# Projecting the last two row blocks of each group tile of tokens by tile of tokens, in a fused attention and two-mixture kernel

## The reference

```
def _moe2_ref(x, domain_probs, w1, w2):      # x 1536 x 512, w1 4 x 512 x 1024, w2 4 x 1024 x 512
    p = domain_probs / (domain_probs.sum(-1, keepdims=True) + 1e-09)
    out = np.zeros((N, D), dtype=np.float32)
    for e in range(E):
        h = np.maximum(x @ w1[e], 0.0)
        out += p[:, e:e + 1] * (h @ w2[e])
    return out.astype(np.float32)
```

## Time and profile before

| | |
|---|---|
| median of 3 runs | 909.2 us (908.07 to 913.29) |
| the profiled execution's own time | 910.04 us |
| its span, first to last instruction | 908.2 us |
| TensorE busy | 860.9 us, 95% |
| weight loads (beside the matmuls) | 695.1 us, 77% |
| VectorE, GpSimd, ScalarE busy | 300.3, 288.8, 221.3 us |
| second mixture, from its first hidden matmul to the end | 378.3 to 908.2 us |
| mean granted TensorE clock over the span | 0.987 of full speed |

### The profile page before, as it was taken

How to read it: one execution, slowest core, us unless ns; L and a number is a source line. 1 busy time by engine, 2 the same in 40 slices (tenths; PEclk the granted TensorE clock), 3 DMA queues, 4 the chain that set the end, 5 groups by cost and what they waited for, 6 DMA issues and landing times.

```text
span 908.2 us, 12900 instructions
## 1 busy us (share of the span) xinstructions
PE 860.9 (95%) x4433; PEld 695.1 (77%) x4434; DVE 300.3 (33%) x776; ACT 221.3 (24%) x476; POOL 288.8 (32%) x162
## 2 busy tenths in 40 slices
PE   7999945999999999999999999999999999999998
PEld 5666623788888788788888888888888888888886
DVE  6777770444444443223121212121212121211212
ACT  4878750033333323311111111111111111111010
POOL 4462613057777778630000650000830001400000
PEclk9999976999999999999999999999999999999999
DMA  6899623146666667620000230000320000001001
GB/s 246 265 315 342 221 78 140 31 124 213 205 204 205 195 220 220 174 94 1 1 0 0 70 116 0 0 0 0 115 71 0 0 0 0 1 0 46 29 17 46
DMA packets 33075, 90.96 MB, mean 100 GB/s; under 512 B 4232, under 2 KB 4616, under 8 KB 33040
## 3 DMA queue, kind: packets, MB, share of 16 engines
q1 hardware_dynamic: 23056, 54.86, 18.1%
q10 hardware_dynamic: 8064, 29.36, 10.6%
q0 software_dynamic: 1920, 6.29, 2.2%
HBM read 72.67 MB, written 17.83 MB: 100 GB/s over the span
## 4 chain that ended last, share of the span: by engine, by line
PE 84%; DMA 8%; DVE 3%; issue 2%; POOL 2%; SPq 1%; ACT 1%; DVEq 0%; ACTq 0%
PE ps L1209 29%; PE ps L1196 29%; PE ps L1153 10%; PE ps L1135 7%; DMA win<-qkv 3%; DMA xg<-x_sorted 3%; PE ps L1008 2%; PE ps L1034 2%; PE ps L1020 2%; POOL x_sorted L473 1%; PE ps L1143 1%; PE ps L1125 1%; PE ps L979 1%; PE ps L1048 1%; ACT arena L528 1%
## 5 line engine op out<-in xcount | busy, mean ns | idle before, releaser
L1209 PE MATMUL ps<-ring,h 128*128 128x512 f32 x1152 | 275.9, 390 | 0.0
L1196 PE MATMUL ps<-ring 128*128 (+1 forms) x864 | 256.4, 389 | 0.0
L278 POOL TENSOR_TENSOR ring<-raw,ring 128x1024 fp32r<-128x1024 f32 x96 | 227.9, 2403 | 84.0 <-ACT ring L273 81.1
L1209 PEld LDWEIGHTS ps<-ring,h 128*128 128x128 f32 x1152 | 215.6, 188 | 44.6
L1196 PEld LDWEIGHTS ps<-ring 128*128 128x128 f32 x864 | 162.1, 188 | 34.0 <-DVE x2b L940 0.2
L947 DVE SCALAR_TENSOR_TENSOR h<-ps,h 128x512 fp32r<-128x512 f32 x96 | 66.3, 691 | 366.3 <-ACT h L597 366.3
L597 ACT ACTIVATE h<-ps 128x512 fp32r<-128x512 f32 x96 | 57.6, 600 | 427.3 <-PE ps L1196 427.3
L273 POOL CAST ring<-raw 128x1024 fp32r<-128x1024 f32 x36 | 38.0, 1055 | 374.8 <-PE ps L1196 320.3
L1196 PE MATMUL ps<-x2b,ring 128*128 (+1 forms) x288 | 112.0, 389 | 0.0
L273 ACT CAST ring<-raw 128x1024 fp32r<-128x1024 f32 x60 | 62.2, 1051 | 176.9 <-PE ps L1153 116.7
L1135 PE MATMUL ps<-ring,xT 128*128 x384 | 91.8, 395 | 0.6 <-DVE xT L900 0.6
(11 more groups left out here) (116 smaller groups left out, 490.2 us busy)
## 6 DMA issues: line engine op xcount, KB each, us to landing
raw<-wts ACTq DMA_DIRECT2D x56, 512.0 KB, 4.2
raw<-wts SPq DMA_DIRECT2D x40, 512.0 KB, 3.8
win<-qkv SPq DMA_DIRECT2D x32, 320.0 KB, 4.1
x_sorted<-ring SPq DMA_DIRECT2D x20, 256.0 KB, 4.9
xg<-x_sorted SPq DMA_DIRECT2D x17, 256.0 KB, 3.4
y_sorted<-yrow SPq DMA_DIRECT2D x16, 256.0 KB, 4.0
win<-qkv SPq DMA_DIRECT2D x8, 384.0 KB, 6.3
result<-xrow SPq DMA_DIRECT2D x12, 256.0 KB, 2.1
```

Source lines behind the costliest of these rows:

```text
L278: nc.gpsimd.tensor_tensor(w_part(u, 1)[:, q * CW:q * CW + CW], raw[:, q, :], w_part(u, 0)[:, q * CW:q * CW + CW].bitcast(F32), ALU.subtrac ...
L1196: ins = nc.tensor.matmul(ps[:, 4 + f % 2, :], w_part(u1, wp)[:, k * F + f * P:k * F + f * P + P], x2T(xp, k)[:, bass.ds(g * 512, 512)], st ...
L1209: ins = nc.tensor.matmul(ps[:, t, :], h2[:, f % 2, hp_, t * P:t * P + P], w_part(u1 + 1, wp)[:, f * DM:f * DM + DM], start=(f == 0 and n = ...
```

## The change

In each group the row blocks 6 and 7 are no longer projected one after the other. project(f) runs for f = 0 to 5 alone, and a new function, finish(), follows the loop. It waits for the split of all 8 blocks and for the fourth quarter of w2. Then, for each tile of tokens, it runs the 3 matmuls of block 6 and the 3 of block 7, and signals y2_ready. hid_used of block 6 is signalled with the last tile. The numbers of matmuls, their operands and the banks are the same. In the loop's passes f = 6 and 7 what is left is hidden(7) and, in the first group, the turning of tiles 10 and 11. No other engine's program is changed.

```diff
--- before.py
+++ after.py
@@ -1214,13 +1214,29 @@
                     if f < KF - 1:
                         ins.then_inc(hid_used, 1)
 
+                def finish():
+
+                    pe.wait_ge(hid_split, n0 + KF)
+                    pe.wait_ge(split_done, 4 * (u1 + 1) + KF // 2)
+                    for t in range(4):
+                        for f in (KF - 2, KF - 1):
+                            for n, (hp_, wp) in enumerate(((0, 0), (0, 1), (1, 0))):
+                                ins = nc.tensor.matmul(ps[:, t, :], h2[:, f % 2, hp_, t * P:t * P + P],
+                                                       w_part(u1 + 1, wp)[:, f * DM:f * DM + DM],
+                                                       start=False, stop=(f == KF - 1 and n == 2))
+                            if f == KF - 2 and t == 3:
+                                ins.then_inc(hid_used, 1)
+                        ins.then_inc(y2_ready, 1)
+
                 hidden(0)
                 for f in range(KF):
                     if f + 1 < KF:
                         hidden(f + 1)
                     if beside:
                         beside(f)
-                    project(f)
+                    if f < KF - 2:
+                        project(f)
+                finish()
 
             for t in range(4):
                 turn_x2(t)
```

## The result

| | before | changed |
|---|---|---|
| median of 4 runs | 910.38 us (908.07 to 913.29) | 933.17 us (931.05 to 936.0) |
| ratio, 95% interval | | 1.0247 (1.0218 to 1.0276) |
| profiled execution, its span | 910.04, 908.2 us | 936.0, 934.2 us |
| TensorE busy | 860.9 us | 867.0 us |
| first hidden matmul of the second mixture | 378.28 us | 382.76 us |

The kernel is 2.5% slower, as forecast. The profiled execution is the slowest of its four runs. Its span is 26.0 us longer, and the first thing to do is to divide that: up to the first hidden matmul, where nothing was changed, it is 382.76 - 378.28 = 4.5 us behind; from there on it is (934.2 - 382.76) - (908.2 - 378.28) = 21.5 us longer. Only the 21.5 belong to the change.

What follows compares the result with a forecast made beforehand. The prediction took gapless TensorE matmuls at full clock to bound the second mixture's stage. Eleven groups at 1.77 us plus 1.93 for the first gave 21.4 us, so 930.6 us, range 927.4 to 936.0.

Steps and rivals of the forecast that it cites:

- The cover: In eleven ordinary groups, block 6's matmuls no longer cover block 7's relu and split: 1.77 us each (1.60 to 2.22).
- The restart: At finish()'s wait, TensorE's first matmul starts 0.17 us after VectorE's low part ends; low end 0.
- The far bound of 0.62: At finish()'s wait, the longest restart considered, with register work behind the wait: 0.62 us after VectorE's end.
- The first group: The group that also turns tiles 10 and 11 of x2, both now before the wait: 1.93 us longer.
- The sum: Over all twelve groups, 11 x 1.77 + 1.93 = 21.4 us added.
- The low end of the sum: Over all twelve groups, the total with an ordinary group at 1.60 us: 19.3 us.
- Order by tiles: In finish(), six matmuls in a row to one bank instead of three, same operands: nothing.
- Earlier accumulations: At each group's end, y2_ready comes 1.36 us apart instead of 0.68: worth nothing inside or at the end.
- hid_used, GpSimd's splits: Waits behind finish(): block 6's later hid_used signal and GpSimd's next split delay nothing.
- Rival B, the clock,: After each of twelve stalls the clock falls, 1.7 us lost each time, total time 951 us; chance 0.04.
- Rivals C and D: C: finish()'s matmuls run faster, 897 us at far bound, chance 0.02. D: other work covers the wait, 909, chance 0.02.

Runs made afterwards that it cites:

- run 1: Changed kernel with block 6 then block 7 order restored, the late wait for block 7 kept: 931.66 us, ratio 1.0223 against the kernel before.
- run 2: Changed kernel with the wait for block 7 moved behind the three matmuls of block 6, tile 0: 923.61 us, ratio 1.0149 against the kernel before.
- run 3: Changed kernel with a third h2 buffer and block 5's projection moved behind hidden(7), tile order kept: 910.58 us, ratio 1.0002 against the kernel before.
- run 4: Changed kernel, two buffers, nine matmuls of block 6 put before the wait for block 7: 910.61 us, ratio 0.9999 against the kernel before.
- run 5: Changed kernel with block 7's low part in two pieces, finish() starting after the first, 128 columns: 928.83 us, ratio 1.0196 against the kernel before.
- run 6: Useless low parts ahead of block 7's: one in changed kernel 957.7 us, three in it 980.14 us, one in kernel before 914.14 us.
- run 7: Changed kernel with a useless low part ahead of block 7's: 128 columns 933.48 us, ratio 1.0257; 256 columns 948.96 us, ratio 1.0438.

## Why the prediction was right, point by point

- **The cover.** As forecast, block 7's chain stands open in each group. The forecast of 1.77 us was 0.02 short of the measured 1.79. Runs 1 to 4 show that the late wait with nothing to run before it is what costs; run 5 that VectorE's low part is a link of the chain, as forecast.
- **The restart.** I took 0.17 us, from one place in the earlier trace rows. In the changed kernel VectorE ends at 652.36 + 0.69 = 653.05. The 24 matmuls last from 653.10 for 5.74 us, the last of them 0.39, so the first counts from 658.45 - 23 x 0.2267 = 653.24: 0.19 us. The far bound of 0.62, with register work behind the wait, did not apply.
- **The first group.** Forecast 1.93, measured 1.84: from the last hidden matmul of block 7 to the last of the group it is 431.90 - 423.65 = 8.25 us, and before it was 425.58 - 419.17 = 6.41. The term was 0.09 too high, mostly because I counted the eleven steps after 422.97 at 0.2267 us although give that piece 3.00 us, 0.12 more than the usual 2.88.
- **The sum.** 11 x 1.79 + 1.84 = 21.5 us, and the stage is 21.5 us longer; forecast 21.4. So good an agreement has some luck in it, since 0.02 us too little in eleven groups and 0.09 too much in the first partly cancel. The low end of the sum is 11 x 1.60 + 1.93 - 0.17 = 19.4 us, not 19.3, which changes nothing. The median, 933.17, is 2.6 above the forecast of 930.6, inside the range. Part of that is the kernel before, whose median over four runs came to 910.38 and not 909.2; the rest is within the interval, in which the difference of the two kernels can be anything from 19.8 to 25.1 us. In the profiled execution another 4.5 us lie ahead of the stage, in code that is the same: over the twelve profiles the first hidden matmul begins anywhere from 376.32 to 382.76 us. One piece of it is seen at 209.57, where a wait for a transfer of tokens left TensorE idle for 2.64 us and the next 24 matmuls took 7.34 us at a mean granted clock of 0.68 over 209 to 213 us.
- **What I costed at nothing.** Order by tiles: shown by runs 1 and 3. Earlier accumulations: run 3 has them and is 1.0002 of before. hid_used, GpSimd's splits: the twelve waits for the low part, 18.0 us, are TensorE's only ones in the stage.
- **Rival B, the clock,** had 0.04. It is right that it did not happen: the granted clock over the stage is 1.00. But the reason given, a single gap of 2.05 us after which the clock stayed, was weak: with 1.82 us in each group it fell in seven of eleven, and with 2.09 us two of eleven were spared. The chance should have been larger, and that the changed kernel stays 0.20 us or more short of those spells is in part luck. The Trainium skill, TensorE: Matmul & The Clock Gate, section "A second HAM failure mode: psum-queue depth-cycling", warns of short idle spells between groups of matmuls; runs 6 and 7 agree with it from 1.82 us up, and the spells of 1.49 and 1.69 us do not.
- **Rivals C and D** fell. The matmuls of finish() are no nearer: 24 of them take 5.44 us in run 3, where no wait stands before them, as those of L1209 do in the earlier trace rows, and in the changed kernel the accumulations follow one another by 1.37 us for six matmuls. And the wait is there.

## What to carry to other kernels

When one engine runs without a gap, the work between a producer's start and its product's first use is a cover with a length: add up the chain that it hides (here 1.83 us and 0.19 for a restart, less the 0.23 of the last matmul itself, 1.79) and compare that with what would still run (here 2.72 us, then nothing). A reordering that puts several inputs behind one wait makes all of them as late as the latest; waiting for each at its first use helps only by the work that stands before that use. In the full order by tiles that was three matmuls, and 1.11 us a group stayed open (run 2). Nothing stayed open once nine matmuls stood there, at the price of part of the new order (run 4), or twelve, at the price of a third buffer (run 3). And finishing results earlier is worth nothing unless someone waits for them, so look for that waiter first.

## What the runs showed of the hardware that was not expected

The cost of an idle spell has a step in it. In these runs up to 1.69 us of idle TensorE in each ordinary group cost the spell alone. At 1.82 us the granted clock fell in 7 of 11 groups, from the 2.4 GHz level to the 1.2 GHz level, and each fall added 1.6 us to the next 24 matmuls. At 3.28 us it fell in every group, and in four of 11 it added 2.6 us or more. The fall can come up to 1.5 us after TensorE has started again, so it is looked for behind the gap as well as in it. In the same program groups with equal spells differ, so a single gap that did no harm, like the one of 2.05 us near the start of the kernel before, is no proof. Whether that gap was spared for the work around it or for its place in time was not tried.
